# Attention written out with two score buffers and one bank for turned rows, and work moved out of the first expert tile

## What is computed

```python
f = 1.0 / (1.0 + np.exp(-f_logit))
for t in range(S):                                   # per batch and head
    state = f[t][:, None] * state + outer(k[t], v[t])
    y[t] = q[t] @ state
logits = x @ w_gate + modality_bias[modality_id]     # x: (3072, 384)
e_idx = argmax(logits); gate = softmax(logits)[e_idx]
out = gate * (relu(x @ w1[e_idx]) @ w2[e_idx])       # w1 384x1024, w2 1024x384
xn = out / rms(out) * rms_g
result = (silu(xn @ w_gate2) * (xn @ w_val)) @ w_out # inner width 1536
```

## Time and profile before

| | |
|---|---|
| median of 3 runs | 866.95 us |
| the profiled execution: time, span | 866.84 us, 865.1 us |
| TensorE busy | 833.0 us, 96% of the span |
| VectorE, ScalarE, GpSimd busy | 55%, 45%, 19% |
| mean granted TensorE clock | 0.988 |
| attention / experts / last stage, about | 0 to 160, 160 to 409, 409 to 865 us |
| read from DRAM, written | 76.75 MB, 19.29 MB |

### The profile page before, as it was taken

How to read it: one execution, slowest core, us unless ns; L and a number is a source line. 1 busy time by engine, 2 the same in 40 slices (tenths; PEclk the granted TensorE clock), 3 DMA queues, 4 the chain that set the end, 5 groups by cost and what they waited for, 6 DMA issues and landing times.

```text
span 865.1 us, 15457 instructions
## 1 busy us (share of the span) xinstructions
PE 833.0 (96%) x5332; PEld 762.5 (88%) x5332; DVE 471.8 (55%) x773; ACT 389.6 (45%) x750; POOL 165.6 (19%) x165
## 2 busy tenths in 40 slices
PE   6999999779999999989999999999999999999997
PEld 6798988779999999989888888888888898888887
DVE  7989898687766666653444333334333333433332
ACT  5988786375666555653423411331241133123112
POOL 5444352318554000000000200100020010001001
PEclk9999999889999999999999999999999999999999
DMA  9877666497988797750200200100020000000000
GB/s 182 188 148 169 150 146 210 153 387 239 301 258 260 245 344 255 255 147 20 74 1 1 74 0 1 66 8 0 0 73 0 0 28 8 0 0 36 0 0 36
DMA packets 44082, 96.49 MB, mean 112 GB/s; under 512 B 9168, under 2 KB 25040, under 8 KB 43920
## 3 DMA queue, kind: packets, MB, share of 16 engines
q1 hardware_dynamic: 39952, 85.81, 33.6%
q0 software_dynamic: 3840, 9.47, 3.1%
q10 hardware_dynamic: 256, 0.79, 0.4%
HBM read 76.75 MB, written 19.29 MB: 111 GB/s over the span
## 4 chain that ended last, share of the span: by engine, by line
PE 78%; issue 2%; DVE 1%; POOL 0%; ACT 0%; DVEq 0%; ACTq 0%
PE h_ps L1779 16%; PE h_ps L1781 15%; PE h_ps L1780 15%; PE ym_ps L1779 7%; PE ym_ps L1781 7%; PE ym_ps L1780 7%; PE xTm_ps L1780 3%; PE xTm_ps L1779 3%; PE xTm_ps L1781 3%; PE xT_ps L1796 1%; PE xTm_ps L1787 1%; POOL out L1443 0%; DVE h_lo L1691 0%; DVE w_lo L1664 0%; ACT w_hi L1461 0%
## 5 line engine op out<-in xcount | busy, mean ns | idle before, releaser
L1754 DVE TENSOR_TENSOR gs<-h_ps,sig 128x512 f32<-128x512 f32 x72 | 49.8, 691 | 175.5 <-ACT sig L1555 175.5
L1555 ACT ACTIVATE sig<-h_ps 128x512 f32<-128x512 f32 x72 | 43.1, 598 | 158.9 <-PE h_ps L1781 158.9
L1566 ACT CAST h_hi<-hid 128x512 fp32r<-128x512 f32 x72 | 44.6, 620 | 150.2 <-DVE hid L1757 150.2
L1779 PE MATMUL h_ps<-x_hi,w_hi 128*128 128x256 f32 x312 | 89.7, 287 | 7.7 <-DVEq L1682 5.1
L1781 PE MATMUL h_ps<-x_lo,w_hi 128*128 128x256 f32 x312 | 89.3, 286 | 0.0
L1780 PE MATMUL h_ps<-x_hi,w_lo 128*128 128x256 f32 x312 | 89.1, 285 | 0.0
L1779 PE MATMUL h_ps<-w_hi,wg_hi 128*128 128x512 f32 x216 | 85.5, 396 | 0.0
L1781 PE MATMUL h_ps<-w_lo,wg_hi 128*128 128x512 f32 x216 | 84.6, 392 | 0.0
L1781 PE MATMUL h_ps<-w_lo,wv_hi 128*128 128x512 f32 x216 | 84.2, 390 | 0.0
L1780 PE MATMUL h_ps<-w_hi,wv_lo 128*128 128x512 f32 x216 | 84.0, 389 | 0.0
L1779 PE MATMUL h_ps<-w_hi,wv_hi 128*128 128x512 f32 x216 | 84.0, 389 | 0.0
(11 more groups left out here) (222 smaller groups left out, 1890.0 us busy)
## 6 DMA issues: line engine op xcount, KB each, us to landing
w_raw<-in_w SPq DMA_DIRECT2D x52, 384.0 KB, 5.0
w_in<-in_w SPq DMA_DIRECT2D x52, 384.0 KB, 5.1
qkf_in<-in_qkf SPq DMA_DIRECT2D x43, 288.0 KB, 5.0
y_sorted<-x_group SPq DMA_DIRECT2D x13, 384.0 KB, 3.4
v_in<-in_v SPq DMA_DIRECT2D x24, 192.0 KB, 4.3
x_regions<-zero_row SPq DMA_DIRECT2D x12, 384.0 KB, 2.9
x_group<-x_regions SPq DMA_DIRECT2D x12, 384.0 KB, 3.9
g_in<-in_wg SPq DMA_DIRECT2D x3, 768.0 KB, 8.1
```

Source lines behind the costliest of these rows:

```text
L1555: nc.scalar.activation(sig[:], g_ps, ACT.Sigmoid).then_inc(sig_done, 1)
L1566: nc.scalar.copy(h2_hi[:, fb % HELD], hid[:]).then_inc(h2_hi_done, 1)
L1754: nc.vector.tensor_tensor(gs[:], g_ps, sig[:], ALU.mult).then_inc(gs_done, 1)
L1779: nc.tensor.matmul(out, hi, rhs_hi, start=first, stop=False)
```

## The change

- `steps` is written out: no loop, no conditions.
- `sc_ps` has two halves, used by turns; TensorE's wait for the mask in front of the scores goes back by one tile, and the mask of m-2 is waited for in front of the growth and the values of m-2.
- `x_ps` is one bank. The product of m-3 waits for the logits of m-4, where it waited for those of m-5.
- `rt_ps` moves into unused columns of the bank of `ds_ps`. So TensorE waits, before it counts at the end of round b = 3, for `grown` of m-2, and before the growth of round b = 0 for `place_sums`, the two instructions of `place` that read `rt_ps`, which VectorE now does before the mask.
- Keys, ks, state and growth use 112 (ROWS) partitions and columns instead of 128; the copy of yT 112 partitions.
- Tiles 20 to 23 have no keys turned and no copy of them; growth, `grown` and `state` stop at tile 19 (growth and `grown` ran to tile 21).
- `pick` runs once, in chunk 5. The picked expert's weights are loaded before the last two v tiles.
- Behind the last chunk the order changes: tile 23 is read into the bank of `ks_ps`, its turned rows into that of `yT_ps`, the picked rows are turned one round earlier, and the hi and lo parts move forward.
- In tile 0 of the experts the semaphore counts of SyncE come before its loads, all of w2's hi parts come first, and `count` comes half-way through hidden(0). Lo of the last w1 part moves into this tile. `rows_of_tiles` goes to the end of tile 0, `shifted_scores` to the end of tile 1, `rows_of_tokens` of tile 2, `gates_of_tokens` of tile 3. The thirds' hi parts go to the ends of tiles 1 to 6, one a tile, and GpSimd sends the tokens behind the last three thirds, eight a time. `wo` is loaded in tile 8 instead of 7. In the last tile the squares come behind the first hidden part's hi, and the sigmoid's table is loaded there.

```diff
-        sc_ps = ps("sc_ps", [P, 2, PR, P])
+        sc_ps = ps("sc_ps", [P, 2, 2, PR, P])
-        x_ps = ps("x_ps", [P, 2, 512])
-        rt_ps = ps("rt_ps", [P, 3, E])
+        x_ps = ps("x_ps", [P, 512])
+        rt_ps = ds_ps[:, DM:DM + 3 * E].rearrange("p (i e) -> p i e", i=3)
...
+                    if b == 0 and c > 1:
+                        dve.wait_ge(counted, c - 1)
+                        rt.place_sums(nc, dve, rt_ps[:, 0], rt_ps[:, 1], marks, (c - 2) * Routing.PLACED)
                     keep = tri[:].rearrange("p (o t) -> p o t", o=1).broadcast_to([P, H, P])
...
+            def read(c, b, t, acc):
+                cc, s, n = t
+                pe.wait_ge(masked, n + 1)
...
+                if n < GROWN and n > 0:
+                    if b == 0 and c > 1:
+                        pe.wait_ge(marks, (c - 2) * Routing.PLACED + Routing.CHOSEN + 2)
+                    growth(s, n)
...
-                    wait_past(pe, masked, n)
+                    wait_past(pe, masked, n - 1)
...
-                    wait_past(pe, x_kept, n - 1)
+                    if n < NT - 1:
+                        wait_past(pe, x_kept, n)
...
                     pe.wait_ge(rt_made, RT_MADE)
+                    pe.wait_ge(grown_done, min(c * B + 2, GROWN))
                     pe.wait_ge(marks, (c - 1) * Routing.PLACED + Routing.CHOSEN)
                     rt.count(nc, rt_ps[:, 0], rt_ps[:, 1]).then_inc(counted, 1)
...
+                        if place == "first" and g == 0 and i == 1:
+                            pe.wait_ge(marks, Routing.CHOSEN)
+                            rt.count(nc, pre_ps, cnt_ps).then_inc(counted, 1)
...
                 if place == "first":
-                    rows_of_tokens()
-                    gates_of_tokens()
+                    rows_of_tiles()
+                if place == "middle":
+                    with dve.If(j < 4):
+                        with only(dve, j, 1):
+                            shifted_scores()
+                        with only(dve, j, 2):
+                            rows_of_tokens()
+                        with only(dve, j, 3):
+                            gates_of_tokens()
```

More of the change, by code:

```diff
@@ L338, in attention, with steps @@
         ahead_sems = Ahead.Sems(nc, ctx, "")
[L339 to L351, removed]
+        xT_ps = sc_ps[:, 0].rearrange("p a j t -> p (a j t)")[:, 0:KD * TM].rearrange("p (k t) -> p k t", k=KD)
+        def steps(step):
+            for c in range(CH):
+                for b in range(B):
+                    step(c, b, c % 2)
             for b in range(B):
-                step(CH, b, 0, None)
+                step(CH, b, 0)
         def tile(c, b, back):
@@ L542, in step @@
                 if (t := tile(c, b, -1)) and not (at(c, 0) and b == 0):
-                    with ahead(b, 1, more):
-                        neg_logs(*t)
-                if t := tile(c, b, 1):
+                    neg_logs(*t)
+                if (t := tile(c, b, 1)) and t[2] < GROWN:
                     _, s, n = t
@@ L558, in step @@
                     last.then_inc(state_done, 1)
+                if at(c, CH) and b == 1:
+                    first.hi_x(nc, act, xT_ps, ahead_sems)
+                    kept(tile(c, b, 2), ks_ps)
+                    first.hi_w1(nc, act, 3, ahead_sems)
                 if t := tile(c, b, 3):
@@ L589, in _ @@
                 neg_logs(0, b, b)
[L590 removed]
+            steps(step)
         @block.vector
@@ L654, in step @@
                 if b == 0 and not (at(c, 0) or at(c, 1)):
-                    dve.wait_ge(counted, c - 1)
-                    rt.place(nc, dve, c - 2, half, rt_ps[:, 0], rt_ps[:, 1], marks, (c - 2) * Routing.PLACED)
-                    if half and not at(c, CH):
-                        first.pick(nc, dve, rt, ahead_sems, (c - 3) * (Ahead.PICKED // 2))
+                    rt.place_rows(nc, dve, c - 2, half, marks, (c - 2) * Routing.PLACED)
+                    if c == CH - 1:
+                        first.pick(nc, dve, rt, ahead_sems, 0)
                 if at(c, CH) and b == 0:
@@ L1478, in _ @@
             act.sem_inc(x_hi_done, 1)
-            hi_w2(0, 0)
+            for g in range(GR):
+                hi_w2(0, g)
             def body(j, place):
@@ L1493, in next_w2 @@
                         hi_w2(j + 1, g)
+                hi_h(0)
+                if place != "first":
+                    next_w1(0)
                 if place == "last":
@@ L1540, in body @@
                 next_w2(3)
-                if place == "first":
-                    hi_third(1)
                 if place == "middle":
-                    with act.If(j < 2 * KD):
-                        for i in range(EARLY, 2 * KD):
-                            with only(act, j, i - 1):
+                    with act.If(j < 2 * KD + 1):
+                        for i in range(2 * KD):
+                            with only(act, j, i + 1):
                                 hi_third(i)
+                                if i == 1:
+                                    act.wait_ge(shifted, 1)
+                                    nc.scalar.activation(prob, biased, ACT.Exp).then_inc(exp_ready, 1)
             used = tiles(act, body)
@@ L1824, in body @@
                 hidden(0)
-                if place == "first":
-                    pe.wait_ge(marks, Routing.CHOSEN)
-                    rt.count(nc, pre_ps, cnt_ps).then_inc(counted, 1)
                 hidden(1)
```

202 lines of the change are left out of this document (95 added, 107 removed).

## The result

The changed kernel takes 887.54 us (median of 4 runs, 882.17 to 890.39), the kernel before 868.01 on the same chip (4 runs): a ratio of 1.0206 [1.0139, 1.0273]. Forecast were 861.6 us and a range of 850 to 870. A second set of runs gave 888.36 and 1.0242 [1.0178, 1.0306]. The profiled execution took 890.39 us (span 888.6), 23.5 more than that of before (866.84, span 865.1).

What follows compares the result with a forecast made beforehand. PE alone was taken to bind two thirds of the span, with the attention nearly balanced between PE, DVE and ACT. Terms -2.6 + 3.4 - 0.7 - 1.5 - 3.7 - 1.5 + 1.7 - 0.3 = -5.2 took 866.84 to 861.6 us, range 850 to 870.

Steps and rivals of the forecast that it cites:

- Clock: Attention: two falls of the granted clock counted behind the four new PE waits, +3.4 us, bounds 0 and 6.8.
- rival of the clock rule: Waits of 1.5 to 2.5 us always drop the clock: four falls (+3.4), one in tile 1 (+1.6): 866.6 us; chance 0.12.
- count wait: Round b = 3, chunks 1 to 4: PE waits for `grown` before counting, 8.8 us in all, bounds 6 and 10.5.
- Narrow tiles: Attention's growth and state reading: narrower loads save 0.2 us a round, bounds 0 and 0.24, making rounds 5.37 us.
- One x bank: Attention's x product: no wait in plain rounds, 1.2 us behind `pick`; rival of 0.3 us in 17 rounds, 866.7, chance 0.17.
- the first six rounds: Attention before round 6: 0.3 us gained, since the wait there is for DVE's token bias.
- second wait on the shared bank: Slower rival: growth of round b = 0 waits 1.9 us for `place_sums` in four chunks, 7.6 us, 872.6 total; chance 0.11.
- End of the attention: From round 24's start to `place` giving rows: 4.4 us becomes about 3.75, -0.7; the 10.7 us behind it unchanged.
- tiles 0 to 2: First expert tiles: shorter PE waits give -1.5 (bounds 0 and -4), -3.7 (-2.1 if the clock falls) and -1.5 us.
- Moved behind tiles 1 to 3: DVE work moved to expert tile ends: `shifted_scores` and `gates_of_tokens` +0.2, `rows_of_tokens` +1.5, together +1.7 us.
- The tokens: GpSimd's token transfers in the experts: no cost, as they are wanted only in the last tile, 100 us later.

Runs made afterwards that it cites:

- filled waits: Nine unneeded key-tile turns before each of four count waits: 863.88 us (0.9968) on the changed kernel with experts mended, 876.95 us (1.0105) on the changed kernel itself.
- two of the kernels: Changed kernel with the third at tile 2's end and later ones moved one tile, 880.63 us; changed kernel with one score buffer, counts in growth's bank, 874.51 us.
- Undoing the trade of banks: Changed kernel with one score buffer, a bank of its own for the counts, one x bank: 866.58 us (1.0004), the second time 864.78 us (0.9961).
- mending the experts as well: Changed kernel with tokens sent by fours, no third at tile 2's end, one score buffer, own bank for counts, one x bank: 861.55 us (0.9932).

## Why the prediction was wrong

**Clock: the step that failed first.** I counted two falls for four waits of 1.5 us and more, at 1.7 us each. All four were followed by one. The windows from 54.1 to 61.1 and from 132.5 to 140.5 show 0.76 and 0.79, 1.7 us lost in each; the one from 80 to 87 shows 0.52 and the one from 107 to 115 shows 0.57, 3.4 us lost in each: 10.2 in all, where the sum had 3.4. The single fall of the earlier trace rows was a short one, and I took its size for all. The rival of the clock rule had the four falls at 0.12, at that same size. The filled waits show the price of the falls, 5 to 11 us in the whole time. The Trainium skill (TensorE: Matmul & The Clock Gate, section on the clock gate) says that an idle TensorE goes back to half its rate, which I had beside that rival. The traces agree with it in direction, not in every wait: 7 of the 8 waits in two of the kernels passed without a fall, and 2 of the 4 before the growth.

**The count wait** was there, in the chunks named, and none in chunk 5: 5.8 us where I had 8.8, just under my bound of 6. I let VectorE's phase move by twice the shortening and took its lateness in the round of the count from the earlier trace rows. In chunk 2 of the changed kernel kT starts 2.62 us behind PE's round (3.01 in the earlier trace rows) and `grown` ends 4.18 behind kT (4.59 there), as the running sum takes 1.23 instead of 1.64. All four chunks wait alike, 1.46, which is the 1.5 that I had for chunk 1 alone.

**Narrow tiles**: 5.37 us rounds as forecast. What I didn't see is that VectorE can take it back: with a single score buffer and one x bank it took most of it in two of three chunks.

**One x bank**: the plain rounds had room and the pick's wait was 0.74 where I had 1.2, but I gave the first six rounds -0.3 and they took +4.0. Their waits for the logits are 0.91 and 1.51 us, where before has 0.44 and 1.59 for masks; two banks don't change them. The rest differs from one execution to the next: round 6 starts at 41.16 us in this profile and at 35.92 in the second one of the same kernel, and with the attention of before at 37.13, 38.50 and 41.27. So the +4.0 can't be put down to the change.

**The second wait on the shared bank**, my slower rival, isn't in the changed kernel. It appears at once when the count moves behind the scores: the bank makes PE wait for VectorE once a chunk, at the one edge or the other. That was the rival's real content, and I gave it 0.11.

**End of the attention, tiles 0 to 2**: -0.6, -1.1, -3.8 and -0.8 against -0.7, -1.5, -3.7 and -1.5. These steps held, with the wait of about 1 us in tile 1 (0.93) that was named; the others, 1.03 and 0.84 us around the end of tile 0 and 0.81 in tile 2, were not in the sum.

**Moved behind tiles 1 to 3**: `rows_of_tokens` was costed at its own 2.6 us from before, where nothing stood beside it. In the changed kernel it ran beside a third on GpSimd and took 5.7; the wait became 5.07, with 6.8 us at 1.2 GHz from its middle on. GpSimd's three subtractions take 3.75 us, 1.25 each, and each of the stretched instructions lasts about as long as one of them. I had read just this stretch in the earlier trace rows (0.95 us that took 4.84) for tile 2, and credited its end, without asking what the moved step would meet. The Trainium skill (SBUF — State Buffer, section on the two separate sides) says that VectorE and GpSimd share a pair of ports that one of them holds for a whole instruction while the other is blocked, among other cases when VectorE's instruction has two inputs in SBUF and GpSimd's reads SBUF. Two of the three stretched instructions have two inputs, and the lengths agree: 1.20 and 1.36 us beside subtractions of 1.25.

**The tokens** were costed at nothing because their result is wanted 100 us later. That asked who waits for the transfers, and not what else is delayed. Of the 23.5 us 13.1 are there, and 8.0 in the second profile of the same kernel. No profile with four in a row has the loss, but those with eight in a row and one score buffer don't have it either; the mechanism stays open.

In sum, most gains of the change came where they were forecast. The clock's falls and tile 3 were taken too small, and the loss of tiles 6 to 8 was left out. Undoing the trade of banks returns the kernel to before's time; mending the experts as well gives 0.9932 [0.9912, 0.9952].

## What to carry to other kernels

Here a bank shared by the work of two engines made PE wait mostly 1.4 to 1.6 us at one of its edges in each chunk, and moving the operation moved the wait. A wait of 1.5 us on PE should be priced with the clock behind it, here mostly 1.7 to 3.4 us more; if it can't be removed, matmuls that do nothing are worth trying in it. Before an operation is moved into a gap, look at what the other engines do there, not only at how long the gap is.

## What was not expected of the hardware

Small VectorE instructions, 0.24 to 0.36 us by themselves, took 1.2 to 1.4 beside GpSimd's subtraction. Thirty-six useless turns made a kernel 11.4 us faster. And the same experts' code took 13 or 8 us more, or nothing more, according to the attention ahead of it, with transfers in rows of eight. The pauses of 1 to 2 us in the last stage's matmuls stand beside transfers of an instruction queue; those of 0.55 and 0.42 us in tile 6 of the changed kernel, in its two profiles, don't, so they may well have another cause.
